# Attention and two MLPs on one core: the first MLP's steps placed between the jobs of the last 22 heads, in chunks of 256 tokens

## The reference, cut to what matters

```python
# q, k, v: (4, 8, 576, 64), 32 heads in all
q_rot, k_rot = rotate(q), rotate(k)                  # cos/sin of the position, halves of 32
scores = (q_rot @ k_rot.T) / sqrt(64)                # 576 x 576 for each head
attn = exp(scores - max); attn = attn / (sum(attn) + 1e-9)
x = (attn @ v) -> (2304 tokens, 512)
h = x @ w_in;  g = s * relu(h)**2 + b;  x = g @ w_out          # first MLP: 512 -> 2048 -> 512
h = x @ w2_in; g = h * sigmoid(1.702 * h); out = g @ w2_out    # second MLP, same sizes
```

## Time and profile before

| | us |
|---|---|
| median of 3 runs (lowest, highest) | 1200.41 (1200.24, 1201.61) |
| the profiled execution | 1201.61 |
| its span, first to last instruction | 1201.6 |
| PE busy | 1157.1 (96%) |
| DVE busy | 596.4 (50%) |
| ACT busy | 584.1 (49%) |
| POOL busy | 218.5 (18%) |
| chain that ended last | PE 85%, ACT 7%, issue 5%, DVE 2% |

### The profile page before, as it was taken

One profiled execution on the slowest core, in us unless ns is written; L12 is line 12 of the kernel. 1 busy time (PEld: TensorE's weight loads), 2 busy tenths in 40 slices (PEclk: granted clock), 3 DMA queues, 4 the chain that ended last, 5 costly groups with the idle time before them and its releaser, 6 DMA issues.

```text
span 1201.6 us, 19306 instructions
## 1 busy us (share of the span) xinstructions
PE 1157.1 (96%) x6576; PEld 1054.0 (88%) x6576; DVE 596.4 (50%) x954; ACT 584.1 (49%) x1146; POOL 218.5 (18%) x310
## 2 busy tenths in 40 slices
PE   3999999999998999999999999999999999999998
PEld 3777887787786999999899999999999999999997
DVE  3788888888886653333233334653332322323222
ACT  3888989989986543323222234542222222223222
POOL 5466576566541000000000000000000000000000
PEclk9999999999998999999999999999999999999999
DMA  4322232232230430000000001320000000000000
GB/s 112 83 67 65 71 75 58 68 75 65 65 86 18 130 99 2 1 1 1 2 1 1 1 1 53 123 71 1 27 1 1 27 1 26 0 26 0 27 1 27
DMA packets 66437, 46.78 MB, mean 39 GB/s; under 512 B 30672, under 2 KB 55888, under 8 KB 66384
## 3 DMA queue, kind: packets, MB, share of 16 engines
q1 hardware_dynamic: 66384, 46.03, 14.0%
HBM read 31.85 MB, written 4.72 MB: 30 GB/s over the span
## 4 chain that ended last, share of the span: by engine, by line
PE 85%; ACT 7%; issue 5%; DVE 2%; DMA 0%; SPq 0%; ACTq 0%; DVEq 0%
PE hps L732 33%; PE acc L756 33%; PE psum L506 7%; PE psum L483 4%; ACT E L542 4%; PE psum L493 4%; PE psum L530 2%; ACT out_rest L563 1%; ACT EThi L549 1%; PE psum L517 1%; DVE ETlo L602 1%; DVE negmax L595 1%; ACTq L43 0%; DMA Klo<-Klo 0%; DMA kraw<-in_k_dram 0%
## 5 line engine op out<-in xcount | busy, mean ns | idle before, releaser
L732 PE MATMUL hps<-xlo,Whi 128*128 128x384 f32 x768 | 257.3, 335 | 1.8 <-issue 1.8
L732 PE MATMUL hps<-xhi,Whi 128*128 128x384 f32 x768 | 257.9, 336 | 0.6 <-issue 0.6
L732 PE MATMUL hps<-xhi,Wlo 128*128 128x384 f32 x768 | 257.8, 336 | 0.0
L732 PEld LDWEIGHTS hps<-xlo,Whi 128*128 128x128 f32 x768 | 144.2, 188 | 6.2 <-issue 2.2
L732 PEld LDWEIGHTS hps<-xhi,Whi 128*128 128x128 f32 x768 | 144.4, 188 | 5.2 <-issue 0.9
L732 PEld LDWEIGHTS hps<-xhi,Wlo 128*128 128x128 f32 x768 | 144.1, 188 | 0.0
L493 PE MATMUL psum<-id_sb,E 128*128 128x128 f32 (+1 forms) x800 | 134.1, 280 | 9.9 <-ACT E L542 7.2
L595 DVE TENSOR_REDUCE negmax<-psum 128x1 f32<-128x576 f32 (+1 forms) x160 | 120.4, 754 | 42.3 <-PE psum L483 41.1
L493 PEld LDWEIGHTS psum<-id_sb,E 128*128 128x128 f32 (+1 forms) x800 | 97.2, 141 | 49.5 <-issue 27.4
L834 ACT ACTIVATE ghi<-act,sb_sb 128x384 fp32r<-128x384 f32 x96 | 59.2, 617 | 157.8 <-PE acc L756 149.5
L858 DVE SCALAR_TENSOR_TENSOR glo<-act,sb_sb,ghi 128x384 fp32r<-128x384 f32 x96 | 59.5, 619 | 145.9 <-ACT ghi L834 145.9
(11 more groups left out here) (66 smaller groups left out, 1897.4 us busy)
## 6 DMA issues: line engine op xcount, KB each, us to landing
wraw<-in_moe_w_in_dram SPq DMA_DIRECT2D x32, 256.0 KB, 2.7
wraw<-in_moe_w_out_dram SPq DMA_DIRECT2D x32, 256.0 KB, 3.0
Khi<-Khi SPq DMA_DIRECT2D x32, 144.0 KB, 2.3
Klo<-Klo SPq DMA_DIRECT2D x32, 144.0 KB, 2.5
out_dram<-xT SPq DMA_DIRECT2D x6, 768.0 KB, 3.5
qraw<-in_q_dram SPq DMA_DIRECT2D x32, 128.0 KB, 2.2
kraw<-in_k_dram SPq DMA_DIRECT2D x32, 128.0 KB, 2.2
vraw<-in_v_dram SPq DMA_DIRECT2D x32, 128.0 KB, 2.0
```

What stands on the lines that cost most here:

```text
L732: mm = pe.matmul(ps[:, 0:CH], w[i][:, kt * P:(kt + 1) * P], piece(x[par][:], kt), start=(kt == 0 and j == 0), stop=(kt == KT - 1 and j == 2))
```

## The change

- The hardware loops are gone: every instruction of all heads and chunks is written out.
- Chunks have 256 tokens (9 of them), so a step of the first MLP is 24 matmuls of 256 columns, one of the second 12 of 256 and 6 of 512.
- Heads 0 to 9 run by lists like those before (`*_ALONE`). From head 10 on, other lists (`*_BESIDE`) put four MLP steps between the jobs of each head: `H` and `G` are the two halves of an H step, `Y` and `Z` those of a Y step, and `relu`, `sq`, `ghi`, `glo` the four operations between them. In this stretch attention has two of the four PSUM buffers (`BESIDE_SLOT`: one for X, PV and B, one for S and prep); H has the third, Y the fourth.
- 22 heads x 4 steps are 88 of the first MLP's 144 steps; the other 56 and the second MLP follow.
- All transposes are of 128 rows and 128 columns; E has a padded end for it.
- Weight tiles of the first MLP are split one by one during attention, hi on ACT, lo on POOL. The odd ones go to DRAM (`wd`, 1 MB each, hi and lo) and come back through two buffers (`ring`) for chunks 0 to 5, two tiles for each head; before chunk 6 they are loaded to stay.
- The attention result goes to DRAM (`xd`) after each pair of heads, and x comes back by chunk (`load_x`, 512 KB); between the MLPs it goes through DRAM too (`yd`). POOL splits it (two instructions of 1024 columns).
- V is rounded on POOL (was ACT), `rest` is taken out by DVE (was ACT). A first exponential at the start of ACT's program comes before any head.

```diff
-    CH = 384
+    CH = 256
     NCH = TOK // CH
+    START_MLP = 10
+    RINGED = 6
+    PE_BESIDE = [order("Z0@-1 Y1@-1 Z1@-1 prep@2 PV0@-1 PV1@-1 PV2@-1 PV3@-1 PV4@-1 H0@0 S1@1 X0@0 Y2@-1 G0@0 Z2@-1 "
+                       "B@-1 H1@0 S2@1 X1@0 H2@0 G1@0 G2@0 S3@1 X2@0 H3@0 Y3@-1 Z3@-1 S4@1 X3@0 Y0@0 G3@0 Z0@0 S0@2"),
...
+    BESIDE_SLOT = {"X": 0, "PV": 0, "B": 0, "S": 1, "prep": 1}
...
+        def ring_load(sp, r, part):
+
+            e = r % 2
+            left = (r - 2) // ODD * NF + 2 * ((r - 2) % ODD) + 2
+            if r < 2:
+                sp.wait_ge(w_stored[e], 16 * (ODD // 2))
             else:
...
+                sp.wait_ge((h_done, y_done)[part], left)
+            sp.dma_start(ring[e][:, 2 * part:2 * part + 2, :].bitcast(F32),
+                         wd[r % ODD, :, 2 * part:2 * part + 2, :]).then_inc((ring_in, ring_out)[part][e], 16)
...
+        def split_x(pool, C):
+            pool.wait_ge(x_in, 16 * (C + 1))
+            need(pool, h_done, NF * (C - 1))
+            pool.tensor_tensor(xhi[C % 2][:], xraw[:], zero[:, :].unsqueeze(2).broadcast_to([P, KT, CH]), ALU.add).then_inc(x_hi, 1)
+            pool.wait_ge(x_hi, C + 1)
+            pool.tensor_tensor(xlo[C % 2][:], xraw[:], xhi[C % 2][:].bitcast(F32), ALU.subtract).then_inc(x_lo, 1)
...
+                for t in range(NT):
+                    a, b = cols(t)
+                    mm = pe.transpose(ps[:, a:b], E[h % 2][:, t * S + j * P:t * S + (j + 1) * P], id_sb[:])
+                mm.then_inc(x_t, 1)
...
+                    store_x(s - 2)
+                    if before_mlp:
+                        load_qk(s + 4)
...
+                    if s == START_MLP - 1:
+                        for r in range(2):
+                            ring_load(sp, r, 0)
+                            ring_load(sp, r, 1)
+                    if of_chunk == PER_HEAD - 1 and 0 <= C + 1 < RINGED:
+                        load_x(sp, C + 1)
```

More of the change, by code:

```diff
@@ L40, in need, with order @@
 def need(eng, sem, value):
-    if not isinstance(value, int) or value > 0:
+    if value > 0:
         eng.wait_ge(sem, value)
[L46 to L58, removed]
+def order(text):
+    toks = []
+    for t in text.split():
+        t, ahead = t.split("@")
+        part = t[-1].isdigit()
+        toks.append((t[:-1] if part else t, int(t[-1]) if part else 0, int(ahead)))
+    return toks
 def fused_kernel(nc, q, k, v, w1_in, w1_out, w_s, w_b, w2_in, w2_out,
@@ new lines, in fused_kernel, with program, run @@
+    POOL_BESIDE = [order("V@1 vlo@0 add@-1"),
+                   order("rot@2 vlo@0 V@1 rot@3")]
+    SLOTS = [int(c) for c in "0231023102311203120312031"]
+    PAIRED = ("B", "invb", "finish", "add")
+    STEPPED = ("H", "G", "relu", "sq", "ghi", "glo", "Y", "Z")
+    LIMIT = {"S": START_MLP, "max": START_MLP, "prep": START_MLP + 1}
+    FIRST, LAST = -5, NHEAD + 4
+    def program(alone, beside, ops, after=None):
+        done = set()
+        def run(s, toks):
+            for kind, j, ahead in toks:
+                h = s + ahead
+                if kind in STEPPED:
+                    h = PER_HEAD * (h - START_MLP) + j
+                    j = 0
+                    if not 0 <= h < STEPS:
+                        continue
+                elif not 0 <= h < NHEAD or (kind in PAIRED and h % 2 == 0):
+                    continue
+                if (kind, h, j) not in done:
+                    done.add((kind, h, j))
+                    ops[kind](h, j)
+        for s in range(FIRST, START_MLP):
+            run(s, [t for t in alone if s + t[2] <= LIMIT.get(t[0], NHEAD)])
+            if after:
+                after(s)
+        for s in range(START_MLP - 4, LAST):
+            run(s, beside[s % 2])
+            if after and s >= START_MLP:
+                after(s)
+        return done
@@ new lines, in H_step @@
+        def H_step(pe, n, half):
+            C, i = n // NF, n % NF
+            w = tile(C, i)
+            if half == 0:
+                wait_weights(pe, C, i, 0)
+                if i == 0:
+                    pe.wait_ge(x_lo, C + 1)
+                if n == 0:
+                    freed(pe, before["H"])
+                need(pe, first_done, n - 1)
+                if C >= NCH:
+                    need(pe, g_done, n - 1)
+            for kt in range(half * KT // 2, (half + 1) * KT // 2):
+                for j, (part, x) in enumerate(((0, xhi), (0, xlo), (1, xhi))):
+                    mm = pe.matmul(hps(n), w[:, part, kt * P:(kt + 1) * P], x[C % 2][:, kt, :],
+                                   start=(kt == 0 and j == 0), stop=(kt == KT - 1 and j == 2))
+            if half:
+                mm.then_inc(h_done, 1)
@@ L586, in attention_scalar @@
[L586 to L588 removed]
+                    act.wait_ge(prep_t, h + 1)
+                    need(act, s_done, NT * (h - 1))
+                    act.copy(Khi[h % 2][D:P, :], row(banks("prep", h))[D:P]).then_inc(k_hi, 1)
+                act.wait_ge(cleared, 1)
@@ L800, in fused_kernel @@
[L800 to L813 removed]
+                    done = attention_tensor(pe)
```

998 lines of the change are left out of this document (503 added, 495 removed).

## The result

| | us |
|---|---|
| before, in the same runs: median of 4 (lowest, highest) | 1200.47 (1200.24, 1201.61) |
| after: median of 4 (lowest, highest) | 1228.59 (1227.46, 1231.33) |
| ratio, 95% interval | 1.0236 (1.0216 to 1.0255) |
| span of the profiled execution | 1226.1 |
| forecast | 1170 (1140 to 1208) |

What follows compares the result with a forecast made beforehand. PE was taken to bound the MLPs and nearly attention. MLP start 148.7, attention 187, matmuls 810.4, waits beside heads 13, chunk 6 3, second-MLP weights 2 and the end 5.5 sum to 1169.6: forecast 1170 us, range 1140 to 1208.

Steps and rivals of the forecast that it cites:

- PE's need and the padding: In attention, 128-row transposes 0.11 us apart cut PE's need from 10.5 to 8.6 us a head; no-gain rival 0.04.
- The gap that the MLP could fill is small (0.6 us for each head): In attention before the change, PE needs 10.5 of 11.1 us a head; padding the transposes is the larger prize.
- I keep 10.7 for each head: Heads 0 to 9, without MLP steps: 10.7 us each, so step 10 begins at 143 us (137 to 148).
- The first chunk's x: From B of heads 6 and 7 to split x: 18.6 us against 13, so H0 waits 5.6, until 148.7.
- K's copies ... cover is the 10 us between k's split and S0: Beside PE work, K's copies, ring loads and stores stay hidden; no term in the sum.
- MLP matmuls: Both MLPs: 256-column matmuls at 0.118 us (0.1155 to 0.121), 810.4 us in all (797 to 826), smaller chunks costing 13.
- Steps beside heads: From head 10, PE stays the bound at 19.9 us a head, with 0.6 us allowed for waits, 13 in all (0 to 44).
- The term of 0.6 us a head: Heads with MLP steps: allowance for PE waiting between X jobs, 13 us in all (0 to 44).
- X chain decides: Rival, chance 0.12: with one buffer for X, PV and B, heads beside MLP steps pass 22.0 us; 1236 at 0.3 a link.
- DVE and POOL take turns: Rival, chance 0.08: beside heads, DVE's two-SBUF-input instructions wait for POOL's; DVE needs 21.2 us a head, total 1185.
- Chunk 6: Before chunk 6, x's load waits in SP's queue behind the last ring load: about 3 us.
- Weights of the second MLP: ACT and DVE split loop about 3.1 us against steps of 2.8: sixteen steps make 5, the two-step lag leaving 2 us.

Runs made afterwards that it cites:

- experiment 1: The kernel before with only the fifth transpose of each X, prep and B group padded to 128 rows and columns: 1180.06 us, ratio 0.9842.
- a later kernel: The three moves, plus chunk 6's x loaded between two ring loads and POOL making the second MLP's lo weights: 1216.93 us, ratio 1.0151.
- the three moves: Changed kernel with `rest` behind k and q on DVE, ACT's weight split mid-step, x ahead of the ring loads: 1208.43 us, ratio 1.0073.
- The last version: The three moves, plus chunk 6's x behind one ring load and DVE's second-MLP weight split one step later: 1204.01 us, ratio 1.0031.

## Why the prediction was wrong

Point by point, by its own steps.

**PE's need and the padding: right.** All transposes are 0.109 us apart, forecast 0.11, and the padding alone gave 20.4 us. "The gap that the MLP could fill is small (0.6 us for each head)" holds for the kernel before, and by it there was nothing to win: the forecast itself priced the smaller chunks at 13 us, which is all of 22 x 0.6. With the padding the gap is 1.9 us a head (8.6 of 10.45), 41 us in all, and the mixing could be worth its price.

**"I keep 10.7 for each head": the step that failed most.** Between heads 2 and 8 a head took 13.4 us; at X0 of head 9 that made 14.3 us more than the sum had. I added up each engine's instructions, saw POOL at 10.0 and ACT at 10, and took the largest sum as the time of a head. None of them set it: the engines were 74 to 80% busy. What set it was ACT's split at the border (it takes 1.06 us, and waits for its load) and `rest` ahead of k and q. Moved together, these gave back 1.7 of the 2.6 us over the 10.83 of experiment 1; the last 0.9 us stays open. The forecast had a term for work that was added, and none for where in the list it was put.

**The first chunk's x: its path was priced nearly right, and PE waited for something else.** From B (142.9) to the split x (164.5) it took 21.6 us, forecast 18.6; x's load took 11.0 us in place of my 3 + 6.4. But H 0 began only at 168.3, and no wait of PE for x is in the trace. "K's copies ... cover is the 10 us between k's split and S0" was wrong: the copies stood behind 2.5 MB of ring and x in one queue. And the exponential that `prep` waited for stood behind ACT's two weight splits, whose loads stood in the same queue. PE's waits between 146 and 180 us:

```profile
PE psum L678 <- DMA Klo<-Klo: 5.2, 1, 5.2
PE psum L723 <- ACT E L740: 4.5, 1, 4.5
```

Timelines of POOL (x's two splits), then of ACT:

```profile
160.14 1.89 POOL L349 TENSOR_TENSOR xhi<-xraw,zero 128x1024 fp32r<-128x1024 f32 x1 [8.30 <-DMA xraw<-xd]
162.11 2.36 POOL L351 TENSOR_TENSOR xlo<-xraw,xhi 128x1024 fp32r<-128x1024 f32 x1
...
163.38 1.05 ACT L294 CAST W<-wraw 128x1024 fp32r<-128x1024 f32 x1 [9.26 <-DMA wraw<-in_moe_w_out_dram]
164.83 1.04 ACT L294 CAST W<-wraw 128x1024 fp32r<-128x1024 f32 x1 [0.40 <-DMA wraw<-in_moe_w_out_dram]
...
166.40 0.73 ACT L740 ACTIVATE E<-psum,negmax 128x576 f32<-128x576 f32 x1
```

Landing times of the issues between 140 and 165 us (KB each, median us), against medians of 2.3 and 2.5 for these copies in the kernel before:

```profile
Khi<-Khi SPq DMA_DIRECT2D x1, 144.0 KB, 9.3
Klo<-Klo SPq DMA_DIRECT2D x1, 144.0 KB, 11.2
```

With the three moves H 0 came at 149.1, where the forecast had it, but by luck: X0(9) came 3.4 us later than forecast (135.7 for 132.3), and the seam was 3.1 us shorter (13.3 for 16.4).

**MLP matmuls: 0.120 us and not 0.118**, inside the bounds given, but 5184 of them: 10 us, and 1 for the 512-column ones. The whole price of smaller chunks is 5184 x 0.120 - 3456 x 0.1733 = 23 us, not 13. The Trainium skill's formula ("TensorE: Matmul & The Clock Gate", section "Wait — 56ns, not 53.3ns?") gives an estimate of 109 ns for 256 columns; the trace has 120.

**Steps beside heads: nearly right.** A head took 20.96 us (461.1 / 22), forecast 20.5, of which 0.2 is the matmul price. The term of 0.6 us a head came out as 1.1: 461.1 less 187 and 2088 x 0.120 is 23.5. PE's waits there are 11 us in 440, 0.5 a head; the rest I put down to the ends of bursts, which count as busy. The rival "X chain decides" did not come: it asked for more than 22.0.

**"DVE and POOL take turns": the mechanism was right, and its price was wrong for this place.** DVE lost 61 us to it, 33 of them beside heads, and still PE hardly waited. It decided only in a later kernel and where I had not looked, in a ring of waits.

**Chunk 6: 3 us forecast, 13 measured** (H 88 to H 100: 48.3 in the changed kernel, less 12 x 2.88 and 0.5 for B). PE's waits of 6.0 and 1.8 stood there, and behind the longer one the granted clock was 0.64 from 664 to 668 us, with matmuls of 256 columns 0.21 us apart in place of 0.12. The queue that I had seen, x behind the last ring load, was the right one, mis-sized; POOL's two splits (1.9 and 2.3 us) stood uncovered behind the load.

**Weights of the second MLP: 2 us forecast, 7 measured** (steps 128 to 149: 70.3 us in the changed kernel, 63.0 by their columns). "The two-step lag hides most" was wrong: a lag hides one late step, not sixteen in a row.

**The balance.** Of the 57.6 us that the sum lacked, 14.3 lie in heads 0 to 9, 5.3 in the seam, 11 in the price of matmuls, 10.6 beside heads, 10 at chunk 6 and 5 at the second MLP's weights: 56.

The last version (1204.0) against the kernel before with padding (1180.1): smaller chunks +23; heads 0 to 9 and the seam +9 (H 0 at 148.2, X0(10) at 139.6); second MLP's weights +8; chunks 5 and 6 +8 (H 88 to H 100 42.7, less 12 x 2.88 and 0.5 for B); less what the mixing gave, 17 (463.2 from H 0 to H 88, against 22 x 10.45 + 2088 x 0.120 = 480.5); less 6 that the padded kernel loses itself (803.0 us from its 22 heads' end to its last matmul for 798.5 of columns, and 5.5 behind it for 4.3): +25, for 24 measured. Mixing heads and MLP steps did fill PE's idle time, as meant, but less than half of the 41 us, and 23 were paid for the chunks that it needs.

The range went wrong for the same reason: its upper end came from one rival, and each small term (10.7 a head, 3, 2, 0.118) had only its middle in the sum, though nearly every error in such a term makes a schedule slower. The upper ends that the text itself named (148 for 143, 826 for 810, 44 for 13) together give 1169.6 + 5 + 16 + 31 = 1222.

## What to carry to other kernels

Price first what a rearrangement can win at most (here PE's idle time from start to start, 41 us, of which 17 were won) against what its tile size costs (23 us); a free repair of the same idle time (padding the transposes, 20 us) may be hidden inside. An engine's sum of busy time is no bound for a pipeline in which every engine follows a fixed list: look, for each instruction added, at what is queued behind it and whether it can stand there waiting for a load. And test suspects in pairs: two parallel waits hide each other, so a repair alone can read as worthless (0 and 1.0 us a head here, 1.7 together).

## What the runs showed of the hardware

- A DVE instruction with two SBUF inputs, or a `tensor_scalar` of only 5 columns, that starts while POOL is in an instruction ends just after it (0.28 and 0.03 us behind it as a rule): 478 ns became 2084 on average, 160 ns became 1480 in one case. DVE instructions with an input in PSUM kept their times (751, 424 ns).
- Taking some of this blocking away in attention gained nothing measurable (EPS removed: 1227.2 for 1228.6); in 22 MLP steps it cost 14 us (84.9 for 70.7).
- A change between 128 and 64 rows costs PE about 0.1 us; with all transposes at 128 rows the kernel before takes 20.4 us less.
- 144 KB copies landed after 9 to 11 us when 2.5 MB stood ahead of them in the queue, and after 2.3 and 2.5 (medians of the kernel before) without.
- The granted clock was 1.00 up to 158 us, 0.54 and 0.50 in PE's waits of 5.2 and 4.5 us, and 0.50 still from 166 to 174 us, where matmuls of 256 columns started 0.21 us apart in place of 0.12: a wait at a seam costs more than its length.
